# Table reads ahead, half of a weight split moved, and a list computed later, in a fused attention, expert and mixing kernel

## The reference, cut to what matters

```python
    attn_out = _attn_ref(**attn_kwargs)
    B, H, S, D = attn_out.shape
    x = np.ascontiguousarray(attn_out.transpose(0, 2, 1, 3)).reshape(B, S, H * D)
    x = _moe_ref(x=x, **moe_kwargs)
    return _moe2_ref(x=x, **moe2_kwargs)

def _moe_ref(x, w_gate, w_local, w1, w2):
...
            h = np.maximum(x[b, s] @ w1[e], 0.0)
            out[b, s] = p[e] * (h @ w2[e])

def _moe2_ref(x, w_theta, w_tok_r, w_tok_i, w_ch):
    theta = x @ w_theta
    cos_t, sin_t = (np.cos(theta), np.sin(theta))
    zr = x * cos_t
    zi = x * sin_t
    yr = np.einsum('ts,bsd->btd', w_tok_r, zr)
    yi = np.einsum('ts,bsd->btd', w_tok_i, zi)
    y = yr + yi
    u = x + y
    return (u + np.maximum(u @ w_ch, 0.0)).astype(np.float32)
```

## Time and profile before

| | us |
|---|---|
| median of three runs | 446.08 |
| the profiled execution | 445.69 |
| its span | 443.8 |
| TensorE busy in it | 412.3 (93%) |
| VectorE busy | 254.1 (57%) |
| ScalarE busy | 194.0 (44%) |

### The profile page before, as it was taken

One profiled execution on the slowest core, in us unless ns is written; L12 is line 12 of the kernel. 1 busy time (PEld: TensorE's weight loads), 2 busy tenths in 40 slices (PEclk: granted clock), 3 DMA queues, 4 the chain that ended last, 5 costly groups with the idle time before them and its releaser, 6 DMA issues.

```text
span 443.8 us, 8201 instructions
## 1 busy us (share of the span) xinstructions
PE 412.3 (93%) x2791; PEld 332.4 (75%) x2792; DVE 254.1 (57%) x403; ACT 194.0 (44%) x428; POOL 78.2 (18%) x128
## 2 busy tenths in 40 slices
PE   7789997299999999999999979999998999999897
PEld 3577786167888888888887758888886788888785
DVE  4888886876363624372116466566668455544253
ACT  1767995614265536363237474433330433112020
POOL 3676784121001111111120011500000000000000
PEclk9989999579999999999999989999999999999999
DMA  8999512918343520627130005500000000000012
GB/s 300 410 424 406 228 55 105 405 55 305 147 155 128 206 78 24 236 86 292 30 112 24 13 20 181 143 0 2 0 0 1 24 25 0 24 25 25 24 49 95
DMA packets 12541, 53.96 MB, mean 122 GB/s; under 512 B 1504, under 2 KB 1632, under 8 KB 10848
## 3 DMA queue, kind: packets, MB, share of 16 engines
q1 hardware_dynamic: 7680, 40.46, 23.5%
q0 software_dynamic: 2960, 9.70, 7.2%
q10 hardware_dynamic: 1872, 3.41, 2.0%
HBM read 40.46 MB, written 13.11 MB: 121 GB/s over the span
## 4 chain that ended last, share of the span: by engine, by line
PE 69%; DVE 8%; ACT 3%; issue 2%; ACTq 1%; POOL 1%; DVEq 0%; POOLq 0%
PE ps L1270 14%; PE ps L1272 14%; PE ps L1271 14%; PE ps L1419 6%; PE ps L1421 6%; PE ps L1420 6%; PE ps L1353 2%; PE ps L1318 2%; PE ps L1277 1%; PE ps L1265 1%; PE ps L1168 1%; ACT w_h L648 1%; DVE ang_r L1041 1%; DVE r_ol L925 1%; DVE z_f L1052 1%
## 5 line engine op out<-in xcount | busy, mean ns | idle before, releaser
L1419 PE MATMUL ps<-z_h,mix_h 128*128 128x512 f32 x144 | 56.8, 394 | 0.0
L1421 PE MATMUL ps<-z_h,mix_l 128*128 128x512 f32 x144 | 56.1, 390 | 0.0
L1420 PE MATMUL ps<-z_l,mix_h 128*128 128x512 f32 x144 | 56.1, 389 | 0.0
L1270 PE MATMUL ps<-w_h,hT_h 128*128 128x512 f32 x104 | 42.6, 410 | 3.6 <-DVE hT_l L977 3.3
L958 DVE TENSOR_TENSOR w_l<-w_raw,w_h (+1 forms) x32 | 37.2, 1219 | 11.9 <-ACT w_h L648 10.9
L592 ACT ACTIVATE p<-s,nmax 128x120 f32<-128x120 f32 x96 | 36.5, 385 | 12.1 <-DVE nmax L798 12.0
L1272 PE MATMUL ps<-w_l,hT_h 128*128 128x512 f32 x104 | 41.2, 396 | 0.0
L1271 PE MATMUL ps<-w_h,hT_l 128*128 128x512 f32 x104 | 41.1, 395 | 0.0
L1270 PE MATMUL ps<-w_h,xT_h 128*128 128x512 f32 x96 | 38.5, 401 | 0.6 <-DVE xT_l L971 0.6
L1272 PE MATMUL ps<-w_l,xT_h 128*128 128x512 f32 x96 | 37.4, 390 | 0.0
L1271 PE MATMUL ps<-w_h,xT_l 128*128 128x512 f32 x96 | 37.4, 390 | 0.0
(11 more groups left out here) (223 smaller groups left out, 851.6 us busy)
## 6 DMA issues: line engine op xcount, KB each, us to landing
w_raw<-w SPq DMA_DIRECT2D x8, 2048.0 KB, 9.7
mix_raw<-mix SPq DMA_DIRECT2D x1, 4608.0 KB, 14.0
ys<-zero SPq DMA_DIRECT2D x1, 3328.0 KB, 35.7
ys<-y_sb ACTq DMA_DIRECT2D x13, 256.0 KB, 2.0
kfull<-k_full SPq DMA_DIRECT2D x8, 400.0 KB, 8.9
vpad<-v_pad SPq DMA_DIRECT2D x4, 768.0 KB, 11.9
xd<-x_sb POOLq DMA_DIRECT2D x12, 256.0 KB, 3.0
out<-o SPq DMA_DIRECT2D x12, 256.0 KB, 2.0
```

Of the source, the lines that this page charges most:

```text
L1270: pe.matmul(ps[:, bank, :], a_h[:, k, :], w_h[:, n, :], start=(k == 0), stop=False)
L1419: pe.matmul(ps[:, i, :], w_h, zh, start=(jb == 0 and m == 0), stop=False)
L1420: pe.matmul(ps[:, i, :], w_h, zl, start=False, stop=False)
L1421: mm = pe.matmul(ps[:, i, :], w_l, zh, start=False, stop=(jb == TPB - 1 and m == 1))
```

## The change

Three things are done.

The table entries of tiles n and n+1 are read together, ahead of `hT_copy(n)`, on ScalarE and on VectorE. The splits of both tiles take the registers.

On ScalarE `x2_scale(0)` and `x2_scale(1)` come ahead of `wth_h`. The first half of tile n+1's second weights is split directly behind `product2(n)`, ahead of the y copy of tile n, and that copy stands between `hT_copy(n+1)` and the second half.

On VectorE the five operations that make `X_EXPERT` move behind `xT_copy(1)`.

```diff
@@ scalar
-            def split(t, raw, hi, arrived, done, a=0, b=STEPS):
-
-                place = place_of(t)
-                new = act.value_load(table[0:1, T_NEW, bass.ds(t, 1)], min_val=0, max_val=1)
+            def is_new(t):
+                return act.value_load(table[0:1, T_NEW, bass.ds(t, 1)], min_val=0, max_val=1)
+
+            def split(t, raw, hi, arrived, done, a=0, b=STEPS, place=None, new=None):
+
+                if new is None:
+                    place, new = place_of(t), is_new(t)
                 with act.If(new != 0):
...
             t = act.snap(n3 + 1)
+            place, new = place_of(t), is_new(t)
+            last_place, last_new = place_of(t + 1), is_new(t + 1)
+            w1_last = act.snap(last_place * STEPS + 2 * STEPS)
             hT_copy(t)
-            split(t, w2_raw, w2_h, w2_in, w2_hi)
-            act.wait_ge(w1_split, place_of(t + 1) * STEPS + 2 * STEPS)
+            split(t, w2_raw, w2_h, w2_in, w2_hi, place=place, new=new)
+            x2_scale(0)
+            x2_scale(1)
+            act.wait_ge(w1_split, w1_last)
             act.sem_inc(passed_act, 1)
             act.wait_ge(wth_in, 16)
             act.activation(wth_h[:, :, :], wth_raw[:, :, :], ACT.Copy).then_inc(wth_hi, 1)
-            x2_scale(0)
-            x2_scale(1)
             turned(0)
             turned(1)
             relu(t + 1)
             x2_scale(2)
             act.wait_ge(hp_done, 1)
             act.activation(sine[:, :], half_pi[:, :], ACT.Sin)
+            act.wait_ge(m2_done, t + 2)
+            act.sem_inc(passed_act, 1)
+            split(t + 1, w2_raw, w2_h, w2_in, w2_hi, 0, STEPS // 2, last_place, last_new)
+            hT_copy(t + 1)
             y_copy(t)
+            split(t + 1, w2_raw, w2_h, w2_in, w2_hi, STEPS // 2, STEPS, last_place, last_new)
             t = act.snap(n3 + 2)
-            split(t, w2_raw, w2_h, w2_in, w2_hi, 0, STEPS // 2)
-            hT_copy(t)
-            split(t, w2_raw, w2_h, w2_in, w2_hi, STEPS // 2, STEPS)
             sines(0)
             z_copy(0)
@@ vector
+            split(0, w1_raw, w1_h, w1_l, w1_hi, w1_split)
+            xT_copy(1, xT1_h, xT1_l)
             link(dve.scalar_tensor_tensor(r_ord[:, E:V], r_used[:, E:V], r_last[:, 1:2], r_ord[:, E:V], ALU.add, ALU.subtract))
...
             dve.tensor_tensor(table[0:1, X_EXPERT, 0:V], r_tf[:, 0:V], r_start[:, 0:V], ALU.min).then_inc(experts_ready, 1)
-            split(0, w1_raw, w1_h, w1_l, w1_hi, w1_split)
-            xT_copy(1, xT1_h, xT1_l)
             for i in range(STEPS):
                 split_step(i, i, w2_raw, w2_h, w2_l, w2_hi, w2_split)
...
             t = dve.snap(n3 + 1)
+            place, new = place_of(t), is_new(t)
+            last_place, last_new = place_of(t + 1), is_new(t + 1)
             hT_copy(t)
-            split(t, w2_raw, w2_h, w2_l, w2_hi, w2_split)
+            split(t, w2_raw, w2_h, w2_l, w2_hi, w2_split, place=place, new=new)
...
-            t = dve.snap(n3 + 2)
-            split(t, w2_raw, w2_h, w2_l, w2_hi, w2_split, 0, STEPS // 2)
-            hT_copy(t)
-            split(t, w2_raw, w2_h, w2_l, w2_hi, w2_split, STEPS // 2, STEPS)
+            split(t + 1, w2_raw, w2_h, w2_l, w2_hi, w2_split, 0, STEPS // 2, last_place, last_new)
+            hT_copy(t + 1)
+            split(t + 1, w2_raw, w2_h, w2_l, w2_hi, w2_split, STEPS // 2, STEPS, last_place, last_new)
             z_split(0)
```

More of the change, by code:

```diff
@@ L959, in split_step, with place_of, is_new, split @@
                                   hi[:, bass.ds(i * SW, SW), :].bitcast(f32), ALU.subtract).then_inc(done, 1)
-            def split(t, raw, hi, lo, hi_done, done, a=0, b=STEPS):
-                place = dve.value_load(table[0:1, T_PLACE, bass.ds(t, 1)], min_val=0, max_val=V - 1)
-                new = dve.value_load(table[0:1, T_NEW, bass.ds(t, 1)], min_val=0, max_val=1)
+            def place_of(t):
+                return dve.value_load(table[0:1, T_PLACE, bass.ds(t, 1)], min_val=0, max_val=V - 1)
+            def is_new(t):
+                return dve.value_load(table[0:1, T_NEW, bass.ds(t, 1)], min_val=0, max_val=1)
+            def split(t, raw, hi, lo, hi_done, done, a=0, b=STEPS, place=None, new=None):
+                if new is None:
+                    place, new = place_of(t), is_new(t)
                 with dve.If(new != 0):
```

## The result

| | before | with the change |
|---|---|---|
| median of 22 runs, us | 446.05 | 447.61 |
| lowest, highest | 444.42, 447.81 | 445.24, 449.82 |
| the profiled execution | 445.69 | 447.74 |
| its span | 443.8 | 445.9 |

The ratio is 1.0038, with a 95% interval of 1.0020 to 1.0056: slower by 0.2 to 0.6%. The prediction was 447.8 with a range of 445.2 to 449.8.

A forecast was written before the change was run, and what follows sets the result against it. TensorE was taken to bound the kernel, almost without idle time through the slot tiles. Terms 0.3 - 0.15 = +0.15 gave 446.2 us without the clock; one fall of 1.6 made 447.8, range 445.2 to 449.8.

The forecast's parts named there:

- The reads ahead: ScalarE's four reads before `hT_copy(n)`: `wth_h` and `mix_product(0)` 2.3 us later, with a new TensorE gap of 2.9 us.
- Half of the weights behind the product: Last tile's second-weight split starts right behind `product2(n)`: the 3.31 us gap before `product2(n+1)` shrinks to 1.0, without low clock.
- The z chain: `z_l` of token tile 0 comes later: TensorE waits 2.0 us before the mixing, leaving 0.3 us of loss.
- The clock: TensorE's clock falls once, behind the new 2.9 us gap before `mix_product(0)`, adding 1.6 us; 42% chance.
- The list: Experts' list moved behind `xT_copy(1)` on VectorE: -0.15 us, between -0.6 and +0.3, with `product2(0)` at 108.0 instead of 108.12.
- rival B: Clock falls twice, behind the gap for `wth_split` and the wait for `z_l` of tile 0: 449.4 us; 25%.
- Rival A: No clock fall, as 2.9 us is too short before `mix_product(0)`; the two waits merely exchange: 446.2 us; 20%.
- Rival C: ScalarE's four reads cost nothing, hidden under something unseen; mixing starts at 265.5, 443.6 us in all; 8%.
- Rival D: ScalarE reaches its wait for the product too late; the long gap stays and the new one is added: about 450; 5%.

The follow-up runs named there:

- fill_both: Changed kernel with unread matmuls in both gaps, 11 ahead of `mix_product(0)` and 7 ahead of the mixing: 445.44 us, ratio 0.9995 to the kernel before.
- reads_only: Kernel before with only ScalarE's four table reads for the last two tiles moved ahead of `hT_copy(n)`: 445.26 us, ratio 0.9983.
- ls_first: store_later with VectorE's `r_ls` moved ahead of the experts' list and the split of the second weights: 441.48 us, ratio 0.9900 to the kernel before.
- fill_first: Changed kernel with 11 unread matmuls only in the gap ahead of `mix_product(0)`: 446.51 us, ratio 1.0001 to the kernel before.
- reads_covered: Changed kernel with three ScalarE reads behind `hT_copy(n)` and the scalings, the fourth before the wait for `product2(n)`: 445.24 us, ratio 0.9980 to the kernel before.
- fill_second: Changed kernel with 7 unread matmuls only in the gap ahead of the mixing: 447.70 us, ratio 1.0033 to the kernel before.
- store_later: reads_covered with tile n's y store issued behind the second half of the last weight split: 442.68 us, ratio 0.9925 to the kernel before.

## Why the prediction was right

**The reads ahead.** Forecast: `hT_h` 2.45 to 2.75 us later, `wth_h` and `mix_product(0)` 2.3. Against the store they moved by 2.45, 2.18 and 2.13. Of the four reads only the first was stretched, and little (0.33), so the lower end was right. The new gap is 2.83, forecast 2.9.

**Half of the weights behind the product.** It was worked out without a fall in front of it, and fill_both is that case: the first pair of `w_h` starts at 18.46 behind the store (forecast 255.9 - 237.41 = 18.49), `product2(n+1)` at 22.80 (forecast 22.83, before 23.11), with 0.82 us idle instead of 3.31 (forecast 1.0; the forecast's own rows give 260.52 - 3.31 + 2.3 = 259.5 for TensorE's arrival and not 259.3, so 0.7). In the changed kernel's own profile, with the fall in front, `product2(n+1)` starts at 24.38.

**The z chain.** Forecast: the mixing waits 2.0 us for it, and 0.2 to 0.45 are left over; I took 0.3. The wait is 1.84, and what is left over is 0.04 (fill_both). This term was sized 0.25 too large, 0.17 of it because reads and scalings delayed `mix_product(0)` by 2.13 and not 2.3.

**The clock.** One fall, put at 1.6 from the 24 matmuls of the kernel before: 1.67 at the first gap, 177.9 - 176.2 = 1.7 at the second. It delays what stands behind `mix_product(0)`'s first matmul and not its start, as the forecast had put it (10.83 with and without the fall). Nearly all of the loss is this term: the mixing starts 1.71 later, of which 1.67 are the clock. In the median it is 447.61 - 446.05 = 1.56. Both kernels have one fall in their profiles, so it is the place of the fall that costs. Before, it slowed `product2(n+1)`, beside which the z chain ran and ended at 266.91; without it the mixing could have started only some 0.6 earlier, as reads_only shows (0.58). With the change it slows what stands ahead of the last weight split and the z chain, and all of it is paid.

**The list.** Forecast -0.15, measured -0.1, by the step that was named: `hT_l` behind `r_ls` and ScalarE's exponential. ls_first shows it by taking that step away.

**The rivals.** The mechanisms of the forecast and of rival B (a second fall, behind the wait for `z_l`) both seem to happen, in different executions. By times and mean clocks together the 2.83 us gap brings its fall in most, and the 1.84 us gap in about half, so that some nine of 22 executions took both, where I gave rival B 25%. That the 0.2 us of error is so small is in part luck: the forecast took one fall for every execution, and the median lies in the middle of a mixture of none, one and two, in which two falls are at least as frequent as one. Rival A, no fall, is out as the usual case: the two executions at 0.985 surely ran so, and the whole lowest group is six of 22. Rival C fell: the reads were not covered by anything. Rival D fell: ScalarE waited 8.88 us for the product.

The row from which rival B took its 1.8 us does not carry a rule. The gap of 1.79 us at 20.26 was followed by the low level in the kernel before, but the same place with 1.79 us in reads_only, 1.80 in ls_first, 2.04 in fill_both and 2.17 in fill_first was not.

The Trainium skill, page "TensorE: Matmul & The Clock Gate", section "What's actually happening", table of states, puts the low level behind a stretch of idle time. Two profiled executions here (fill_first and reads_covered) have a fall behind 1.82 us of idle time between long matmuls, the changed kernel none behind 1.84, and reads_only none behind 1.96. So the length of the idle time alone doesn't decide it: the trace agrees that idle time brings the fall, not that a longer one always does.

## What to carry to other kernels

A table read costs its engine little when it stands behind queued work and its full time (here 0.62 us) when it stands ahead of the first instruction of a chain: read early, but under cover. When a wait is moved, ask of each new gap on TensorE whether the clock will hold through it: here a fall added 1.7 us behind a gap of 1.8 or 2.8, and a few unread matmuls in the gap were a cheap test of it. And of several things ordered on one queue, put the store's issue behind whatever starts the next long chain; here that was worth 1.1 us.

## What the runs showed of the hardware

- The granted clock fell behind idle times of 1.82 us in two of three profiled executions with such a gap between long matmuls (1.82, 1.82, 1.84), behind 2.83 and 3.3 in all four, and not behind 1.96 (reads_only) or the shorter ones of the other kernels' last tiles. Among the unprofiled executions some must have kept the full clock behind the long gaps too: by a mean clock of 0.984 or 0.985, 2 of the changed kernel's 22, 3 of fill_second's 12 and 6 of the 81 of the kernel before that were timed beside the experiments. One fall cost 1.7 us.
- Eleven unread 128x512 matmuls held the clock through a gap of 2.8 us (fill_both and fill_first), and delayed what followed by nothing that can be seen (`mix_product(0)` at 10.83 with and without them).
- A table read out of SBUF took 0.28 us on ScalarE's queue in most rows, 0.33 where it was the first of four behind the store's issue, 0.47 once and 0.52 to 0.56 where it was the first behind `hT_h`; in the row of four it was 0.61 to 0.67 from one to the next with the work around it.
- From `product2(0)` to the store it is 129.3 us in each of the eleven profiled executions, but the part before it varies by more than any edit here moved: the store was issued between 236.07 and 240.53 us in the profiled executions of the ten other kernels, and at 237.41 before. I did not look for the cause; the latest one (store_later) has three stretches of low clock in its first 44 us, where the kernel before has one.
